# Full table rows, and the last batch's dense stages in another order, in a fused attention, channel-mix and FFT-mixer kernel

## The reference, cut to what matters

```python
# q, k, v: (4, 8, 576, 64)                                   attention, thresholded
scores = q @ k.T / sqrt(64);  thresh = max(scores) - tau
attn   = softmax(where(scores >= thresh, scores, -1e9));  x = attn @ v    # (4, 576, 512)

x_prev = x shifted by one position                           # channel mix
r = sigmoid((mu_r * x + (1 - mu_r) * x_prev) @ w_r)
k = relu((mu_k * x + (1 - mu_k) * x_prev) @ w_k);  x2 = r * ((k * k) @ w_v)

u  = x2 + real(fft(fft(x2, axis=1), axis=2))                 # Fourier mixer
un = (u - mean(u)) / sqrt(var(u) + 1e-6)
out = u + relu(un @ w_ch1) @ w_ch2                           # 512 -> 2048 -> 512
```

## Time and profile before

| what | us |
| --- | --- |
| median of three runs (lowest to highest) | 1105.21 (1104.08 to 1118.18) |
| the profiled execution | 1105.52 |
| its span, first to last instruction | 1103.7 |
| PE busy in it | 1073.6 (97%) |

### The profile page before, as it was taken

How to read it: one execution, slowest core, us unless ns; L and a number is a source line. 1 busy time by engine, 2 the same in 40 slices (tenths; PEclk the granted TensorE clock), 3 DMA queues, 4 the chain that set the end, 5 groups by cost and what they waited for, 6 DMA issues and landing times.

```text
span 1103.7 us, 18440 instructions
## 1 busy us (share of the span) xinstructions
PE 1073.6 (97%) x7088; PEld 1006.8 (91%) x7088; DVE 564.3 (51%) x1097; ACT 512.7 (46%) x1250; POOL 397.2 (36%) x344
## 2 busy tenths in 40 slices
PE   6999999999999999999998999999999999999998
PEld 6899999998999998999997997888888888888998
DVE  6998765566864466874554753344223223223211
ACT  5988875646875656875655632221111111111110
POOL 5897663433563443562413423331111111111000
PEclk9999999999999999999999997899999999999999
DMA  8634201031301131301114015300200100200000
GB/s 235 182 111 159 57 24 57 26 122 49 99 24 57 43 117 36 100 24 34 40 66 151 1 68 227 120 1 1 69 1 1 69 1 1 68 1 1 36 1 33
DMA packets 37252, 69.31 MB, mean 63 GB/s; under 512 B 4134, under 2 KB 18604, under 8 KB 36140
## 3 DMA queue, kind: packets, MB, share of 16 engines
q1 hardware_dynamic: 36860, 67.80, 19.4%
q10 hardware_dynamic: 304, 0.33, 0.1%
HBM read 55.84 MB, written 12.28 MB: 62 GB/s over the span
## 4 chain that ended last, share of the span: by engine, by line
PE 86%; DVE 7%; ACT 2%; issue 2%; POOL 2%; DMA 0%; SPq 0%; DVEq 0%; ACTq 0%; POOLq 0%
PE PB L737 21%; PE PB L739 20%; PE PB L738 20%; PE PB L794 10%; PE PB L764 6%; PE PB L777 6%; DVE probs L1294 2%; DVE neg_s L1280 1%; POOL fold_l L665 1%; DVE rowinv L1304 1%; ACT mix_v L1098 0%; DMA k_raw<-kT_dram 0%; ACT exps L1027 0%; PE PB L808 0%; PE PB L802 0%
## 5 line engine op out<-in xcount | busy, mean ns | idle before, releaser
L1238 ACT ACTIVATE h_hi<-PB 128x464 fp32r<-128x464 f32 (+1 forms) x80 | 44.4, 555 | 337.9 <-PE PB L739 337.9
L1474 DVE SCALAR_TENSOR_TENSOR h_lo<-PB,h_hi 128x464 fp32r<-128x464 f32 (+1 forms) x80 | 51.0, 638 | 265.8 <-ACT h_hi L1238 265.8
L794 PE MATMUL PB<-v_sb,probsT 128*128 128x64 f32 (+1 forms) x1440 | 177.5, 270 | 0.0
L794 PEld LDWEIGHTS PB<-v_sb,probsT 128*128 128x128 f32 x1440 | 172.1, 192 | 0.0
L1294 DVE SCALAR_TENSOR_TENSOR probs<-neg_s,thresh,exps 128x576 f32<-128x576 f32 x144 | 150.6, 1046 | 0.0
L1036 ACT ACTIVATE probsT<-PB 128x384 f32<-128x384 f32 (+1 forms) x288 | 109.5, 433 | 69.3 <-PE PB L777 67.5
L1280 DVE TENSOR_SCALAR_CACHE_REDUCE neg_s<-PB,taus 128x576 f32<-128x576 f32 x144 | 117.0, 813 | 47.5 <-PE PB L764 43.1
L737 PE MATMUL PB<-un_h,w1h 128*128 128x464 f32 (+1 forms) x320 | 122.6, 383 | 0.0
L739 PE MATMUL PB<-un_h,w1l 128*128 128x464 f32 (+1 forms) x320 | 119.7, 374 | 0.0
L738 PE MATMUL PB<-un_l,w1h 128*128 128x464 f32 (+1 forms) x320 | 119.4, 373 | 0.0
L738 PE MATMUL PB<-h_lo,w2h 128*128 128x464 f32 (+1 forms) x320 | 118.8, 371 | 0.0
(11 more groups left out here) (158 smaller groups left out, 2353.4 us busy)
## 6 DMA issues: line engine op xcount, KB each, us to landing
q_raw<-qT_dram SPq DMA_DIRECT2D x62, 160.0 KB, 3.1
k_raw<-kT_dram SPq DMA_DIRECT2D x64, 144.0 KB, 3.1
w_raw<-w_dram SPq DMA_DIRECT2D x8, 1024.0 KB, 9.1
cs<-cs_scr SPq DMA_DIRECT2D x4, 1740.0 KB, 7.9
u_scr<-x2T SPq DMA_DIRECT2D x4, 1152.0 KB, 5.4
cd<-cd_scr SPq DMA_DIRECT2D x4, 1032.0 KB
v_sb<-v_dram SPq DMA_DIRECT2D x16, 256.0 KB, 2.9
u_in<-u_scr SPq DMA_DIRECT2D x4, 928.0 KB, 5.6
```

The source lines that it names most:

```text
L794: last = nc.tensor.matmul(bank(6 + p)[:, i * DH:i * DH + width], probsT[:, n % 2, kt * P128:(kt + 1) * P128], v_sb[:, kt, pair % 2, p * DH ...
L1474: nc.vector.scalar_tensor_tensor(h_lo[:, ft % 3, 0:w], bank(4 + ft % 3)[:, 0:w], 0.0, h_hi[:, ft % 3, 0:w].bitcast(F32), ALU.max, ALU.subt ...
```

## The change

1. **Full rows.** Table `odd` and the tiles `mid_v`, `mid_h`, `mid_l` get 128 rows instead of one, with zeros in the table's new rows. The third row tile of `y_h` and `y_l` is padded with zeros to 128 rows, and the u matmuls read all 128. In attention the last transpose writes 64 keys instead of 128: its stationary operand narrows from 128x128 to 128x64.
2. **Batch 3's start.** Its x, mix and r steps get slots of their own, and batch 2's sums are made later and through early tiles (`q_cp_early` and so on).
3. **Tables.** `cs` comes in two transfers, cosines first, and two of the four `w_raw` transfers go behind it.
4. **Order of y** in batch 3: the cosine groups' second pairs come first, and their copies with them.
5. **First chunk's steps.** Mean, centring, square, the sums of squares and the split of W2 stand at other places of batch 3.

```diff
-U_AT_DRAIN = [39, 39, 41, 42, 42]
+U_AT_DRAIN = [39, 39, 41, 43, 43]
+X_AT_ALONE = [2, 2, 4, 6, 6]
+MIX_AT_ALONE = [3, 4, 6, 7, 8, 9, 10, 11, 13, 14, 15, 16, 18, 18, 19, 19]
...
 def u_read_at(d, pr):
-    return (40, 43)[pr] if drains(d) else U_AT[2 * pr + 1]
+    return (42, 45)[pr] if drains(d) else U_AT[2 * pr + 1]
 def u_sum_at(d):
-    return 44 if drains(d) else U_AT[2]
+    return 49 if drains(d) else U_AT[2]
+def u_row_at(d):
+    return 50 if drains(d) else U_AT[4]
+def y_order(d):
+    return (0, 2, 4, 1, 3, 5) if alone(d) else range(2 * ST)
...
     if (stage, c) == ("r", 0):
-        return 8 + i
+        return 10 + i * 3 // 4 if alone(d) else 8 + i
...
-                    sp.dma_start(odd[0:1, :], odd_scr).then_inc(cd_in, 16)
+                    sp.dma_start(odd[:, :], odd_scr).then_inc(cd_in, 16)
                     if d == B - 1:
-                        for gi in range(4):
-                            load_w1(gi)
+                        load_w1(0)
+                        load_w1(1)
                     yield 35
                     sp.wait_ge(v_ready, d * 8 + 8)
-                    sp.dma_start(cs[:, :, :, :], cs_scr).then_inc(cs_in, 16)
+                    sp.dma_start(cs[:, :, :, 0:FS], cs_scr[:, :, :, 0:FS]).then_inc(cs_in, 16)
+                    sp.dma_start(cs[:, :, :, FS:2 * FS], cs_scr[:, :, :, FS:2 * FS]).then_inc(sines_in, 16)
+                    if d == B - 1:
+                        load_w1(2)
+                        load_w1(3)
...
+                nc.gpsimd.memset(y_h[ST - 1][:, :].bitcast(F32), 0.0)
+                nc.gpsimd.memset(y_l[ST - 1][:, :].bitcast(F32), 0.0).then_inc(y_padded, 1)
...
                         if stage == "k" and c == 0 and alone(d):
-                            yield MIX_AT[7] + 1
+                            yield 14
+                            pool.wait_ge(u_loaded[0], 16)
+                            nc.gpsimd.memset(mean512[:, :], 1.0 / D)
                             sum_u(0, 0, 1)
...
+                            if alone(d):
+                                pool.wait_ge(x2_ready, d * 8 + 8)
+                                nc.gpsimd.memset(y_l[ST - 1][:, :].bitcast(F32), 0.0).then_inc(y_padded, 1)
...
-                            last = nc.tensor.transpose(bank(4 + unit % 2)[:, (kt - k0) * P128:(kt - k0 + 1) * P128],
-                                                       probs[:, n % 2, kt * P128:(kt + 1) * P128], ident[:, :])
+                            keys = min(P128, S - kt * P128)
+                            last = nc.tensor.transpose(bank(4 + unit % 2)[0:keys, (kt - k0) * P128:(kt - k0 + 1) * P128],
+                                                       probs[:, n % 2, kt * P128:kt * P128 + keys], ident[:, :])
...
-                        nc.tensor.matmul(o, mid_h[0:1, ss], odd[0:1, :].bitcast(F32R), start=False, stop=False)
-                        nc.tensor.matmul(o, mid_l[0:1, ss], odd[0:1, :].bitcast(F32R), start=False, stop=False)
+                        nc.tensor.matmul(o, mid_h[:, ss], odd[:, :].bitcast(F32R), start=False, stop=False)
+                        nc.tensor.matmul(o, mid_l[:, ss], odd[:, :].bitcast(F32R), start=False, stop=False)
...
+                    else:
+                        dve.wait_ge(u_outer, 2 * (B - 1))
...
-                                if alone(d) and c == 0 and ft == 5:
+                                if alone(d) and c == 0 and ft == KFT - 1:
                                     center(0, 0)
-                                if alone(d) and c == 0 and ft == KFT - 1:
-                                    split_w2(0, True)
-                                    split_w2(0, False)
                         if stage == "v":
+                            if alone(d) and c == 0:
+                                yield slot_of(d, "v", 0, 0)
+                                split_w2(0, True)
+                                split_w2(0, False)
```

More of the change, by code:

```diff
@@ L280, in build @@
         at_end = m.at
-        y_l1 = [m.put(f"y_l{st}", [P128, 2 * KC], F32R) for st in (1, 2)]
+        y_l2 = m.put("y_l2", [P128, 2 * KC], F32R)
         gate_alone = Place(at_end).put("gate_alone", [P128, DT, HALF], F32)
@@ L340, in build @@
         u_in = r.put("u_in", [P128, 2, DT, W], F32)
+        early = Place(r.at)
+        q_cp_early = [early.put(f"q_cp_early{i}", [P128, FS], F32) for i in range(2)]
+        diff_early = [early.put(f"diff_early{i}", [P128, FS], F32) for i in range(2)]
+        summ_early = [early.put(f"summ_early{i}", [P128, FS], F32) for i in range(2)]
         cent = r.put("cent", [P128, DT, W], F32)
+        assert early.at <= r.at
         part = r.put("part", [P128, 2, W], F32)
@@ L370, in build @@
         put_un(r, low)
-        assert r.at <= at_ksq and low.at <= m.at
+        assert r.at <= at_ksq and low.at <= top
         w2h, w2_raw, w2l = [[part[i] for part in w2_parts] for i in range(3)]
@@ L432, in gate_of, with sums_of @@
             return gate_alone if alone(d) and c == 1 else gate
+        def sums_of(d):
+            return (q_cp_early, diff_early, summ_early) if drains(d) else (q_cp, diff, summ)
         def add_dft(engine, tile, near, far):
@@ L927, in dense @@
                     if alone(d):
-                        for g in range(2 * ST):
+                        for g in y_order(d):
                             second_pair(d, g)
@@ L1103, in mixing @@
                             act.wait_ge(tables_stored, 80)
-                        if i == 4 and d > 0:
+                        if i == 4 and d > 0 and not alone(d):
                             act.wait_ge(u_inner, d)
@@ L1176, in dense @@
                         act.wait_ge(dft_ready, d * 5 + 2 * pr + 2)
-                        nc.scalar.activation(q_cp[pr][:, :], ring(d, "u", 0, 2 * pr + 1)[:, 0:FS], ACT.Copy).then_inc(qcp_ready, 1)
-                    yield u_at(d)[4] + (2 if drains(d) else 0)
+                        nc.scalar.activation(copy[pr][:, :], ring(d, "u", 0, 2 * pr + 1)[:, 0:FS], ACT.Copy).then_inc(qcp_ready, 1)
+                    yield u_row_at(d)
                     act.wait_ge(dft_ready, d * 5 + 5)
@@ L1182, in dense @@
                     row = ring(d, "u", 0, 4)[0:1, 0:FS]
-                    nc.scalar.activation(diff[0][0:1, :], row, ACT.Copy)
-                    nc.scalar.activation(summ[0][0:1, :], row, ACT.Copy).then_inc(row_copied, 1)
+                    nc.scalar.activation(dif[0][0:1, :], row, ACT.Copy)
+                    nc.scalar.activation(add[0][0:1, :], row, ACT.Copy).then_inc(row_copied, 1)
                 def square(c):
@@ L1415, in dense @@
                     fold(d, 1)
-                    for g in range(2 * ST):
+                    for at, g in enumerate(y_order(d)):
                         st, kind = g // 2, g % 2
                         rows = SROWS[st]
-                        yield Y_AT[g]
-                        dve.wait_ge(yh_ready, d * 6 + g + 1)
+                        yield Y_AT[at]
+                        dve.wait_ge(yh_ready, d * 6 + at + 1)
+                        if alone(d) and st == ST - 1:
+                            dve.wait_ge(y_padded, 2)
                         nc.vector.tensor_tensor(y_l[st][0:rows, kind * KC:(kind + 1) * KC], ring(d, "y", 0, g)[0:rows, 0:KC],
-                                                y_h[0:rows, st, kind * KC:(kind + 1) * KC].bitcast(F32), ALU.subtract).then_inc(yl_ready, 1)
+                                                y_h[st][0:rows, kind * KC:(kind + 1) * KC].bitcast(F32), ALU.subtract).then_inc(yl_ready, 1)
+                    copy, dif, add = sums_of(d)
                     for pr in range(2):
```

106 lines of the change are left out of this document (58 added, 48 removed).

## The result

| | us |
| --- | --- |
| forecast (range) | 1085.7 (1078 to 1093) |
| measured, median of 8 | 1093.61 (1093.28 to 1095.38) |
| the kernel before, median of 8 beside it | 1105.05 |
| after / before | 0.9919 (95% interval 0.9892 to 0.9946) |
| the profiled execution, and its span | 1093.62, 1091.8 |

What follows compares the result with a forecast made beforehand. PE, busy 97% of the span, was taken as the bound. The terms -7.7 -3.2 -1.7 +1.6 +1.6 -11.8 +1.7 sum to -19.5, from the profiled 1105.5 to 1086.0, less 0.3 to the median: 1085.7, range 1078 to 1093.

Steps and rivals of the forecast that it cites:

- Full rows: Beside attention, batches 0 to 2: no row-count switches in u and y groups, 2.6 a batch, -7.7 together.
- Batch 3's start: Batch 3 up to y: waits before k's first group gone, -3.2, and the half clock there, -1.7.
- the walk: Batch 3's ACT, POOL and PE streams followed with row durations: mix 11 late, +1.6; sums of squares' wait 3.4, +1.6.
- the half clock after it: After the wait at the variance in batch 3: one new half-clock stretch, +1.7.
- The narrower transpose: Attention's last transpose: columns of the weights do not set the pace, so narrowing to 64 gives 0; other bound 5.4.
- Rival 2: Attention's transposes: the narrow transpose pays 5.4, time 1080.3; chance 0.10.
- y, u and W1: Batch 3: W1 starts 9.6 earlier after y, and its first stretch saves about 2.2 at full clock; together -11.8.
- The rule on loads and row groups: Trainium skill, at row-count switches: a load overlaps running matmuls only when the row group differs, so full rows give nothing.
- rival 5: u and y groups: full rows give nothing back, the 0.22 steps stay, time 1095.3; chance 0.03.
- Rival 1: Middle of batch 3: no new waits at mix 11 or the sums of squares, no dip, time 1079.1; chance 0.18.
- Rivals 3 and 4: 3: half clock again through u, 1092.8, chance 0.16; 4: half clock from the variance's wait until W1, 1130.7, chance 0.02.
- rival 6: Batch 3's u: the sines come late (2.5), or other small waits, time 1088.2, inside the forecast's own spread.

Runs made afterwards that it cites:

- split_late: The changed kernel with DVE's split of W2's first part moved from beside the sums of squares to behind the scaling; 1090.98.
- rows33: The changed kernel with u's third row tile read on 33 rows again; 1098.58, a single execution.
- odd1: The changed kernel with the odd table's matmuls on one row again; 1095.03, a single execution.
- adds_later: The changed kernel with DVE's first adds of u into x2T one slot later in batches 0 and 1; 1091.96.
- tables_undone: The changed kernel with the table in one transfer behind all four weight transfers and y's sums in the old order; 6 executions, 1095.0 to 1096.3.
- narrow: The kernel before with only the last transpose narrowed from 128x128 to 128x64; ratio to the kernel before 1.0015 (0.9986 to 1.0044).
- sums_first: The changed kernel with POOL's three sums of squares put ahead of mixes 12 to 15; 1086.54, 0.9849 of the kernel before.

## Why the prediction was wrong, step by step

- **The step that failed** is "by the walk the sums end at 632.2. The wait grows to 3.4", with the half clock after it: +7.3 instead of +3.3 (wait +4.8 for +1.6, half clock +2.5 for +1.7), 4.0 of the 7.9 us between forecast and measurement. It named the right wait, and one more mix ahead of the sums is a part of the cause. But the larger part was a term put at nothing: DVE's split of W2 beside the first sum. I took the sum's duration from a row without that subtraction beside it, and noted the subtraction only as no longer ahead of a mix. "split_late" takes 2.6 of the wait away by moving the split alone and leaves 3.98, against my 3.4. The other 0.6 is the walk, which let the mixes 12 to 15 come earlier with PE: the sums began 0.9 after PE arrived ("split_late": 0.4) where the walk had them 0.4 before. The mixes' `mix_h` stands behind the square on ACT, which waits for the centring, which the change moved from k 5 to k 7.
- **Full rows**: the mechanism was right (steps of 0.13, "rows33" and "odd1"), the size too large: -5.3 against -7.7, 1.8 a batch instead of 2.6. I took PE as the bound in u's slots and did not look at whether DVE had a pause there. "adds_later" shows 0.5 of the missing 2.4 on DVE; the rest is open.
- **The narrower transpose**: 0, right, for the reason given. Rival 2 is out. (Its price was off: half of 0.11 in 108 slots is 5.9, not 5.4.)
- **Batch 3's start**: -4.4 against -4.9 and +1.1 against +1.6, right. PE did wait for mix 11, 0.80 where the walk had 1.5.
- **y, u and W1**: -10.4 against -11.8. Full clock, as forecast. Off were the sines, which land at y + 8.8 instead of y + 7 (the upper bound, y + 10, held them) and cost 1.2 of the 1.4; the second fold came at y + 4.0, as forecast. That the clock stayed full was luck as to its reason: I gave the missing wait before u, and in "tables_undone" the wait is back and the clock still full. It goes with the full rows, and my forecast had not asked them for it. By the trace of "narrow", some 7 of these 10.4 us exist only against the slower kind of the kernel before.
- **The rule on loads and row groups**: the trace and "rows33" contradict it; rival 5 is out. Rival 1 did not occur; "sums_first" has its mechanism (no wait at the sums of squares, no dip) but not its time of 1079.1. Rivals 3 and 4 did not occur, nor did rival 6's stall of 2.5: the sines cost one wait of 0.97.
- **What I could not see**: the kernel before has a faster kind of execution at 1098 to 1100, and the profiled one belonged to the slower kind. The first three times (1104.08, 1105.21, 1118.18) did not show it.

## What to carry to other kernels

When a chain of small steps is moved, walk each engine's stream again from its own order: what stands behind the moved step on ACT can be what POOL's next step waits for. Give steps whose reader is near (the sums of squares) the place ahead of those whose reader is 15 us away (the mixes for the second half), and keep DVE's long work on two operands from running when POOL takes up the sum that PE waits for. Zero-pad operands so that the row count does not change inside a PE-bound stream; it costs no columns. And take several executions before pricing a half-clock stretch: the one that was profiled may be of a kind that only some of them show.

## What the runs showed of the hardware

- A change of row count between matmuls of 290 columns (128 to 33 and back) costs about 0.185 us on top of the columns, spread over two steps of 0.23 where the others are 0.135. With such changes a kernel had slower groups of executions (9 of 9 with a wait of 2.19 before u, 7 of 11 without, 9 of 20 in the kernel before), with full rows none did (40 executions, 6 of them with a wait of 2.43 before u).
- POOL and DVE slowed each other by about what was left of the other's work when they began: a POOL sum of 464 columns took 3.20 with 2.18 of a DVE subtraction left, 1.41 with 0.36 left, 1.16 without; a DVE mask took 2.01 with 1.39 of POOL's `k_lo` left, 1.24 with 0.62 left, 0.81 without.
- A table of 1740 KB in pieces of 13920 bytes had landed 7.9 us after its issue, the same table in two transfers with pieces of 1160 bytes 8.6 us after the first one's.
- Narrowing the stationary operand of one transpose in five from 128 to 64 columns shortened the five loads by 0.03 (0.58 to 0.55) and the slots by nothing.
